# A fused attention, experts and MLP kernel: the MLP's gate moved to the head of the next slot, four partial sums of a quarter carried through ScalarE

## The reference, cut to what matters

```python
def _moe2_ref(x, w_in, w_out):          # the last of three stages, "the MLP"
    h = x @ w_in                        # 1536 tokens, 512 -> 2048
    g = h * np.cos(h)                   # the gate
    return (g @ w_out).astype(np.float32)   # 2048 -> 512

def reference(**kwargs):
    attn_out = _attn_ref(**attn_kwargs)     # decayed linear attention, 2 x 8 heads x 768 x 64
    x = attn_out.transpose(0, 2, 1, 3).reshape(B * S, H * D)
    x = _moe_ref(x=x, **moe_kwargs)         # 4 experts, relu, weighted by domain_probs
    return _moe2_ref(x=x, **moe2_kwargs)
```

## Time and profile before

| | us |
|---|---|
| median of 3 runs | 847.24 |
| lowest, highest | 847.1, 850.56 |
| the profiled execution | 849.6 |
| its span (first to last instruction) | 846.3 |
| PE busy in the span | 809.5 (96%) |
| DVE busy | 620.4 (73%) |
| POOL busy | 404.6 (48%) |
| ACT busy | 309.1 (37%) |

### The profile page before, as it was taken

One profiled execution on the slowest core, in us unless ns is written; L12 is line 12 of the kernel. 1 busy time (PEld: TensorE's weight loads), 2 busy tenths in 40 slices (PEclk: granted clock), 3 DMA queues, 4 the chain that ended last, 5 costly groups with the idle time before them and its releaser, 6 DMA issues.

```text
span 846.3 us, 11656 instructions
## 1 busy us (share of the span) xinstructions
PE 809.5 (96%) x4362; PEld 668.7 (79%) x4362; DVE 620.4 (73%) x947; ACT 309.1 (37%) x578; POOL 404.6 (48%) x362
## 2 busy tenths in 40 slices
PE   8999999999999999999999999989998989989896
PEld 7888888888888888888888888866676767667675
DVE  6987766766676676676676676678878787777885
ACT  4643222232222222222222222555554545454532
POOL 4876243343333333333334332487667665766631
PEclk9999999999999999999999999999999999999999
DMA  9832101120111211010110111011010101100003
GB/s 329 312 136 63 38 27 37 38 75 26 38 38 38 63 38 37 26 46 31 36 39 25 38 38 26 1 39 36 26 38 14 43 23 35 38 12 26 0 1 149
DMA packets 19867, 44.83 MB, mean 53 GB/s; under 512 B 2344, under 2 KB 2392, under 8 KB 19812
## 3 DMA queue, kind: packets, MB, share of 16 engines
q1 hardware_dynamic: 19812, 44.10, 16.6%
HBM read 40.93 MB, written 3.17 MB: 52 GB/s over the span
## 4 chain that ended last, share of the span: by engine, by line
PE 65%; DVE 18%; ACT 9%; issue 5%; POOL 1%; DMA 1%; SPq 0%; ACTq 0%; DVEq 0%; POOLq 0%
PE ps L1237 30%; PE ps L1218 27%; DVE temps L1077 6%; DVE temps L1073 3%; ACT temps L785 3%; PE ps L1302 3%; ACT temps L787 2%; PE ps L1295 1%; DVE temps L1055 1%; DVE h_f L1044 1%; ACT temps L768 1%; DVE y L1044 1%; PE ps L1135 1%; DMA att<-att_in 1%; PE ps L1185 1%
## 5 line engine op out<-in xcount | busy, mean ns | idle before, releaser
L510 POOL TENSOR_TENSOR h_lo<-temps,h_hi 128x512 fp32r<-128x512 f32 (+1 forms) x128 | 135.2, 1057 | 295.5 <-ACT h_hi L674 295.4
L674 ACT ACTIVATE h_hi<-temps 128x512 fp32r<-128x512 f32 (+1 forms) x128 | 67.3, 526 | 336.9 <-DVE temps L932 336.9
L915 DVE TENSOR_TENSOR y<-ps,y 128x512 f32<-128x512 f32 x180 | 124.1, 689 | 71.7 <-PE ps L1237 71.7
L1237 PE MATMUL ps<-h_hi,w_hi 128*128 128x512 f32 x384 | 150.5, 392 | 0.1
L1218 PE MATMUL ps<-x_hi,w_hi 128*128 128x512 f32 (+1 forms) x448 | 150.4, 336 | 0.1
L1218 PE MATMUL ps<-x_hi,w_lo 128*128 128x512 f32 (+1 forms) x448 | 150.5, 336 | 0.0
L1218 PE MATMUL ps<-x_lo,w_hi 128*128 128x512 f32 (+1 forms) x448 | 150.5, 336 | 0.0
L1237 PE MATMUL ps<-h_lo,w_hi 128*128 128x512 f32 x384 | 150.3, 392 | 0.0
L1237 PE MATMUL ps<-h_hi,w_lo 128*128 128x512 f32 x384 | 149.4, 389 | 0.0
L563 POOL TENSOR_TENSOR x_lo<-temps,x_hi 128x512 fp32r<-128x512 f32 x55 | 72.7, 1332 | 69.2 <-ACT x_hi L740 69.2
L1218 PEld LDWEIGHTS ps<-x_hi,w_hi 128*128 128x128 f32 x448 | 84.7, 189 | 12.9 <-DVE temps L927 0.3
(11 more groups left out here) (106 smaller groups left out, 1409.2 us busy)
## 6 DMA issues: line engine op xcount, KB each, us to landing
w_raw<-w_in SPq DMA_DIRECT2D x96, 256.0 KB, 2.7
att<-att_in SPq DMA_DIRECT2D x24, 512.0 KB, 7.2
temps<-p_scr SPq DMA_DIRECT2D x4, 768.0 KB, 4.3
out<-y SPq DMA_DIRECT2D x12, 256.0 KB, 2.0
att<-dp_in SPq DMA_DIRECT2D x1, 24.0 KB
p_scr<-att SPq DMA_DIRECT2D x1, 24.0 KB
lam<-lam_in SPq DMA_DIRECT2D x1, 6.0 KB, 1.8
```

The source lines that it names most:

```text
L510: pool.tensor_tensor(hs_lo[side][:, f, at], ring(s, i), f32(hs_hi[side][:, f, at]), ALU.subtract).then_inc(s_hlo, 1)
L674: act.activation(hs_hi[s % SIDES][:, f, at], ring(s, i), ACT.Copy).then_inc(s_hhi, 1)
L915: dve.tensor_tensor(at, from_bank, at, ALU.add).then_inc(s_y, 1)
L1237: mm = pe.matmul(ps[:, DOWN_BANK + g % DOWN_BANKS, :], ww[:, s // SIDES % 2, f, at], hh[side][:, f, tokens], start=(f == 0 and n == 0), st ...
```

## The change

1. On DVE gate v - 1 is no longer behind the add of part 0 in slot v - 1, but at the head of slot v, ahead of the wait for `kf` of v. The differences and the combinations move with their gates, the first into slot 3, the second and third into slot 4. All adds of parts 0, 1 and 2 of slot v + 1 now stand between `r2` of v and gate v. Two of the four adds of the stage before (`down`) move too.
2. The sums of g0, g1, g14 and g16 (`CARRIED`) are no longer added by DVE in quarters 0 to 6. In quarters 1 to 6 ACT first copies the sum from SBUF into the group's bank (`carry_in`, semaphore `s_pre`), PE accumulates onto it (`start` is false), and in quarters 0 to 6 ACT copies the bank back (`carry_out`, semaphore `s_y3`). In the last quarter nothing is carried. Who waits for a bank waits for `s_y3` or `s_y2` by the group that had it (`wait_free`).
3. In the first quarter POOL does the low of gate 0 ahead of the sums of weights, and the low of the next quarter's first weights behind the low of the first difference.
4. In the last quarter an addition of g0 to g7 waits only for the combinations that it needs, not for all seven.

```diff
+CARRIED = (0, 1, 14, 16)
...
 # POOL, first quarter
+                if m == 0:
+                    gate_low(m, 0, 0)
+                    w2_sums(m)
+                    gate_low(m, 1, 1)
+                    w2_sums_low(m)
+                    token_low(m, 2, t2[0])
+                    w1_low(q + 1, 0)
...
 # ACT
+            def carry_in(m, i):
+                if m == 0 or m == FULL:
+                    return
+                wait_free(act, m, i)
+                act.wait_ge(s_y3, carried_count(m - 1, i))
+                act.activation(second_bank(m, i), sum_place(m, i), ACT.Copy).then_inc(s_pre, 1)
+
+            def carry_out(m, i):
+                if m == FULL:
+                    return
+                act.wait_ge(s_dn2, GROUPS * m + i + 1)
+                act.activation(sum_place(m, i), second_bank(m, i), ACT.Copy).then_inc(s_y3, 1)
+
             for v in range(GATES):
                 q, m, j = QUARTERS + v // 6, v // 6, v % 6
+                if j == 1 and m:
+                    carry_in(m - 1, 14)
+                if j == 2 and m:
+                    carry_in(m - 1, 16)
+                if j == 3:
+                    carry_in(m, 0)
+                    carry_in(m, 1)
                 act.wait_ge(s_g, v + 1)
...
+                if j == 1 and m:
+                    carry_out(m - 1, 14)
+                if j == 2 and m:
+                    carry_out(m - 1, 16)
+                if j == 3:
+                    carry_out(m, 0)
+                    carry_out(m, 1)
...
 # DVE
                         if i < 8:
-                            dve.wait_ge(s_comb, 7)
+                            dve.wait_ge(s_comb, (1, 4, 7, 7)[i // 2])
...
+                if v:
+                    gate(v - 1)
+                if m < FULL and j == 3:
+                    dve.wait_ge(s_gate, 6 * m + 3)
+                    token_sum(m, 0, 0, t2[0], gate_of(m, 2), gate_of(m, 0))
+                if m < FULL and j == 4:
+                    dve.wait_ge(s_gate, 6 * m + 4)
+                    token_sum(m, 1, 0, t2[1], gate_of(m, 3), gate_of(m, 2))
+                    token_sum(m, 2, 1, t2[2], gate_of(m, 3), t2[0])
...
                 dve.wait_ge(s_k, v + 1)
...
-                second(v + 1, 0)
...
-                dve.scalar_tensor_tensor(out=gg[:, t, :], in0=cs[:, t, :], scalar=1.0, in1=bank, op0=ALU.subtract,
-                                         op1=ALU.mult).then_inc(s_gate, 1)
...
-                second(v + 1, 1)
-                second(v + 1, 2)
+                for part in range(3):
+                    if v + 1 < GATES:
+                        second(v + 1, part)
+            gate(GATES - 1)
...
 # PE
+                        bank = second_bank(m, i)
+                        if carried(m, i) and m:
+                            pe.wait_ge(s_pre, carried_count(m - 1, i))
+                        else:
+                            wait_free(pe, m, i)
```

More of the change, by code:

```diff
@@ L119, in rotating, with carried, carried_count, added_count @@
     return ROTATING * m + (i if i < at else at + (i - at) // 2)
+def carried(m, i):
+    return m != FULL and i in CARRIED
+def carried_count(m, i):
+    return len(CARRIED) * m + CARRIED.index(i) + 1
+def added_count(m, i):
+    return ADDED * m + (rotating(m, i) - ROTATING * m if m == FULL else i - 2) + 1
+def group_of(r):
+    m, i = min(r // ROTATING, FULL), r - ROTATING * min(r // ROTATING, FULL)
+    at = 8 if m == FULL else 14
+    return m, i if i < at else at + 2 * (i - at)
 def split_done(m, n):
@@ L312, in second_sum, with sum_place, second_bank, wait_free @@
             return own_sums[:, c, :, :] if half is None else y[:, 2 * half:2 * half + 2, chunk(c)]
+        def sum_place(m, i):
+            if i < 14:
+                return second_sum(i // 2)[:, i % 2, :]
+            return y[:, SIDE_D[i - 14], chunk(CHUNKS - 1)]
+        def second_bank(m, i):
+            return ps[:, SECOND_BANK + rotating(m, i) % SECOND_BANKS, :]
+        def wait_free(engine, m, i):
+            r = rotating(m, i) - SECOND_BANKS
+            if r >= 0:
+                mm, ii = group_of(r)
+                if carried(mm, ii):
+                    engine.wait_ge(s_y3, carried_count(mm, ii))
+                else:
+                    engine.wait_ge(s_y2, added_count(mm, ii))
         def w1_split(q, i):
@@ L1061, in combined, with gate @@
                 dve.tensor_tensor(at, one, other, ALU.add).then_inc(s_comb, 1)
+            def gate(v):
+                t = v % T_RING
+                dve.wait_ge(s_sq, v + 1)
+                if v >= T_RING:
+                    was, k = (v - T_RING) // 6, (v - T_RING) % 6
+                    if was < FULL:
+                        if k != 2:
+                            dve.wait_ge(s_glo, split_done(was, (0, 1, None, 3, 7, 8)[k]))
+                        if k < 4:
+                            dve.wait_ge(s_t2, 4 * was + (1, 4, 2, 4)[k])
+                    else:
+                        dve.wait_ge(s_glo, split_done(was, k))
+                dve.scalar_tensor_tensor(out=gg[:, t, :], in0=cs[:, t, :], scalar=1.0, in1=ps[:, v % UP_BANKS, :],
+                                         op0=ALU.subtract, op1=ALU.mult).then_inc(s_gate, 1)
             for v in range(GATES):
@@ L1117, in _ @@
-                second(v + 1, 1)
-                second(v + 1, 2)
+                if v == 1:
+                    down(STEPS - 1, 2)
+                for part in range(3):
+                    if v + 1 < GATES:
+                        second(v + 1, part)
+            gate(GATES - 1)
+            for part in range(3):
+                second(GATES, part)
             second(GATES, 3)
@@ L1324, in second @@
                     else:
-                        r = rotating(m, i)
-                        bank = ps[:, SECOND_BANK + r % SECOND_BANKS, :]
-                        if r >= SECOND_BANKS:
-                            pe.wait_ge(s_y2, r - SECOND_BANKS + 1)
+                        bank = second_bank(m, i)
+                        if carried(m, i) and m:
+                            pe.wait_ge(s_pre, carried_count(m - 1, i))
+                        else:
+                            wait_free(pe, m, i)
+                    opens = m == 0 or not (kept(m, i) or carried(m, i))
                     if m != FULL and i < 14:
@@ L1338, in second @@
                             second_tile(bank, [(hi, h2_hi[:, row, :]), (hi, h2_lo[:, row, :]), (lo, h2_hi[:, row, :])],
-                                        True, True)
+                                        opens, True)
                         else:
-                            second_tile(bank, halves(q, f, at // P + i % 2, row), True, True)
+                            second_tile(bank, halves(q, f, at // P + i % 2, row), opens, True)
                         continue
@@ L1350, in second @@
                     second_tile(bank, halves(q, 0, d, rows[0]) + halves(q, 1, d, rows[1]),
-                                m == 0 or not kept(m, i), m == FULL or not kept(m, i))
+                                opens, m == FULL or not kept(m, i))
             for v in range(GATES + 4):
```

77 lines of the change are left out of this document (33 added, 44 removed).

## The result

| | before | changed |
|---|---|---|
| median of 3 runs, us | 847.24 | 835.12 |
| lowest, highest | 847.1, 850.56 | 834.36, 836.1 |
| profiled execution, its span | 849.6, 846.3 | 836.1, 833.7 |
| ACT busy, us | 309.1 | 334.4 |
| DVE busy, us | 620.4 | 604.5 |

The ratio is 0.985 with a 95% interval of 0.981 to 0.989. The time forecast was 834.5, with 827 to 843 as the range.

What follows compares the result with a forecast made beforehand. No engine is full; DVE's chain in series with ACT's makes PE lose 5.0 us a quarter. Terms -1.8 + 0.6, -9.6, -1.4 and -0.7 give -12.9 us from the 847.2 median: 834.3, said as 834.5, range 827 to 843.

Steps and rivals of the forecast that it cites:

- the walk: One steady quarter of the MLP, reckoned slot by slot from unit costs: 34.75 us, 1.6 less than before.
- the 0.3 before g8: Steady quarter: one of PE's remaining stops, before g8, claimed at 0.3 us.
- the forecast had 0.6: First quarter: a PE that is late there takes back 0.6 us of the gain at the start.
- the waits of 0.76 us before gates: Every slot: DVE's wait for ACT's Sin and Square, 0.76 us, claimed to be gone after the change.
- the `r2` of 1.56 us: DVE, slot 3 to 4 before the change: claimed to end as POOL's `w2s_lo` does (669.92 + 2.69).
- the third rival: ACT becomes the bound, slower: added copies ahead of `kf`, slack 0.4 us in slots 4 and 1; 854 us; chance 0.07.
- 7d - 0.8: Price of d us more on each ACT copy; at d 0.5 a loss of 2.7 us a quarter.
- The first rival: Ports lost at the differences: low of gate 3 starts first, DVE stands about 1.2 us more; 842.5 us; chance 0.14.
- -1.8: Start: `r1` of v = 4 at 568.0 instead of 569.82, by the first gate's low ahead of the sums.
- The moved stop before g3: First quarter: PE's 3.30 us stop before g0 moves to g3, of about 3.6 us.
- -0.7: End, last quarter: split wait for combinations, an add ahead of the gate, PE's stop one group on; 0.7 us less.
- neither saving can be booked alone: Steady quarter: 2.4 us off DVE's adds against eight ACT copies of 4.2 us ahead of `kf`; one quarter walked instead.

Runs made afterwards that it cites:

- e6: Changed kernel with one more ACT copy of 128x512, into unused SBUF, ahead of each copy in and out: 859.8 us, 38.9 us a quarter.
- e1: Changed kernel without the four carried sums, DVE adds g0, g1, g14 and g16 again: 828.5 us, 32.97 us a quarter.
- e2: Changed kernel with gate, differences, combinations and adds back in the old order, four sums still carried by ACT: 858.7 us, 38.02 us a quarter.
- e5: Changed kernel with POOL's old order in the first quarter, sums of weights ahead of the low of gate 0: 836.0 us.

## Why the prediction was right, point by point

**The quarter.** Right in its working. By turns, the walk against the trace: slot 3 to 4 5.8 and 5.70; 4 to 5 5.5 and 5.35; 5 to 0 5.3 and 5.25; 0 to 1 5.1 and 4.98; 1 to 2 5.7 and 5.83; 2 to 3 7.3 and 7.24. It gave 34.75 for 34.35; the 0.4 is spread over five of the turns. PE's stops are nearly where the walk put them: g0 1.0 us (walk 1.1), g3 1.1 (1.3), g9 0.6 (0.7); the 0.3 before g8 isn't there. The walked quarter was taken for all six. The last five repeat within 0.04 us; the first took 35.42, 1.1 more, for which the forecast had 0.6. One sign was not as told: the waits of 0.76 us before gates are gone from slots 0, 3, 4 and 5 (0.34 is left in slot 3), but those of slots 1 and 2 are 1.36, for the adds of g14 and g16 no longer fill them. They cost nothing: behind these gates DVE stands again, 1.54 and 2.07 us, for `kf`. One row was misread on the way: the `r2` of 1.56 us ends at 673.16 and POOL's `w2s_lo` at 672.61, so `r2` did not end with it but ran when it had ended. The walk reckons so.

**The copies' price.** Taken as 0.53 us with a bound of 0.48, measured 0.52 behind a copy from SBUF and 0.48 behind one from PSUM, with 0.58 to 0.60 us for one. Right. The slack that the third rival gave them was wrong (e6): at d = 0.5, the only one run, its 7d - 0.8 gives 2.7 us for the measured 4.5. What was missing is the copy in slot 0, the slack of slot 1, and what a late `r2` loses against POOL.

**The ports.** The first rival named a low of gate 3 that starts ahead of the second difference. That happened nowhere: in the steady quarters the low starts 0.7 us behind it (673.59 for 672.89), and the difference lasts 0.68. In the first quarter the difference does last 1.77 us (the first row), but it meets the lows of weights that part 3 of the change put there (two, from 565.93 to 568.89); the low of gate 3 starts at 568.84.

```profile
567.67 1.77 DVE L1134 TENSOR_TENSOR temps<-temps,h_f 128x512 f32<-128x512 f32 x1
...
741.58 0.68 DVE L1134 TENSOR_TENSOR temps<-temps,h_f 128x512 f32<-128x512 f32 x1
```

So the rule of the Trainium skill, page "SBUF — State Buffer", section "SBUF: two separate sides", was the right way to walk DVE and POOL, and the traces agree with it: whichever comes first keeps the ports, and the other lasts longer by what is left of the first. The pair of before and e1 shows both orders of the same two instructions. Before, POOL's low starts 0.10 us ahead: it lasts 1.31 us and the difference 1.76. In e1 the difference starts 0.10 us ahead: it lasts 0.68 and the low 1.74. So the one race was worth 1.1 us a quarter, and a shift of 0.2 us decided it. No run here moves one of them alone on purpose.

**The start.** -1.8 was forecast, and it was -0.5, both from `r1` of v = 0 and from the span's start. The step that failed is the time of POOL's sums: I had them end 0.4 us later than before, at 559.8; they ended at 560.7. The low ahead of them was done at 557.4 and not near 556.4: it took 1.74 us, and one of the four sums 1.19, since DVE's `r2` of slot 2 and a difference held the ports, so `kf` of slot 3 came at 562.24 and not at 561.3. The rest is the difference of 1.77 us above. The moved stop before g3 was nearly as forecast (3.0 us by the profile, 3.6 in the walk); that PE also stops 1.5 us before g2, and that the clock falls behind the stop before g3 as it did before behind the one before g0, the forecast doesn't say.

**The end.** -0.7 was forecast, and it was +0.6. What the walk says of the stop is right: the add of g0 went ahead of the gate, and PE's stop moved on by one group. The step that failed is to take a gain from it. The combinations stayed between the gate and `r1`, the stop kept nearly its full length (2.0 for 2.1 us), and behind the last stop all waits for the last gate. `r2` of v = 43 met POOL's low (1.39 us, 0.68 before), so `r1` of v = 44 came 6.95 us after `r1` of v = 43 and not 6.24. By `r1` of v = 47 this is made up (25.96 us for 26.0). What is left is `r2` of v = 47, which met POOL's low as well and lasts 1.45 us for 0.87: the last gate comes 4.0 us after `r1` of v = 47 for 3.4, and from PE's next start behind it to the end it is 10.3 us in both.

**The parts.** The sum was right, but the forecast said that neither saving can be booked alone and did not say which part pays. e1 and e2 do: the gate's place is worth 36.36 - 32.97 = 3.4 us a quarter, and the carried sums, put on top, take 1.4 back. Put into the old order they make it slower. The errors at the two ends, +1.3 each, and the ones in the quarters, -2, and in the slots behind them, -0.3, nearly cancel. That the time came within 1 us of the 834.5 is in part luck.

## What to carry to other kernels

When two engines hand a tile to and fro, put the step that waits at the head of the next round, behind the other work that is due anyway: here that gave 3.4 us of 36 a quarter with no instruction less, some 2.3 by filled waits and 1.1 by a race with POOL that was won by 0.1 us in place of lost by as much. Before moving work to an engine because its busy share is low, look at what stands behind the new place in its queue: here ACT was half idle, and eight copies more, 4.0 us of its time, made the quarter 4.5 us longer. And when two stops of PE are merged into one longer one, price the clock behind it too, if PE has nothing more to wait for: then a fall cost 1.6 to 2.6 us, and nothing where another stop followed.

## What the runs showed of the hardware that was not expected

- ACT copied 128x512 float32 from SBUF to PSUM in 0.588 to 0.597 us, from PSUM to SBUF in 0.582 to 0.585, and (e6) from SBUF to SBUF in 0.626 to 0.629. Accumulating matmuls onto what ACT had written cost PE nothing: behind the first they start 0.23 us apart as the others do.
- In the MLP of these kernels PE's clock fell behind every stop of 2.65 us and more by the profile (granted 0.50 to 0.54 behind it, 1.2 GHz), and behind none of 1.73 us or less, unless a longer one followed soon. Between 1.8 and 2.4 us both occur. The changed kernel and e5 have the same last quarter and the same stop of 1.97 us at the same place (23.45 us after `r1` of v = 43), and the clock fell in the first and not in the second. It fell behind 2.36 us in e1 and not in e5. So the length of such a stop doesn't settle it, nor does what PE did in that quarter before it.
- The time until `r1` of v = 0 is 543.3 to 543.9 us in eight of the kernels and 544.7 to 544.8 in five, with the same stages ahead of it. So a difference of 1 us between two of these traces is only safe when it is counted inside the stage.
